# Portions of one lane pair's output between the scores of the next, in a recurrent attention kernel

## The reference

```python
def _attn_ref(r, k, v, w, u):          # B, H, S, D = 2, 8, 768, 48
    state = zeros((B, H, D, D))
    for t in range(S):
        kt, vt, rt, wt = k[:, :, t], v[:, :, t], r[:, :, t], w[:, :, t]
        cur = einsum('bhd,bhe->bhde', u[None] * kt, vt)
        y[:, :, t] = einsum('bhd,bhde->bhe', rt, state + cur)
        state = wt[:, :, :, None] * state + einsum('bhd,bhe->bhde', kt, vt)
    return y
...
x = attn_out.transpose(0, 2, 1, 3).reshape(B, S, H * D)
X = fft(fft(x, axis=1), axis=2);  u = x + real(X)
un = (u - mean(u)) / sqrt(var(u) + 1e-06)
x = u + maximum(un @ w_ch1, 0) @ w_ch2
...                                     # then a gated block with w_in, w_sg, w_out
```

## Time and profile before

| | us |
|---|---|
| median of 3 runs | 447.88 |
| lowest, highest | 446.8, 449.64 |
| the profiled execution | 449.1 |
| its span, first to last instruction | 447.0 |
| TensorE busy in the span | 411.4 (92%) |
| VectorE, ScalarE, GpSimd busy | 257.8, 164.7, 155.2 |

### The profile page before, as it was taken

How to read it: one execution, slowest core, us unless ns; L and a number is a source line. 1 busy time by engine, 2 the same in 40 slices (tenths; PEclk the granted TensorE clock), 3 DMA queues, 4 the chain that set the end, 5 groups by cost and what they waited for, 6 DMA issues and landing times.

```text
span 447.0 us, 10469 instructions
## 1 busy us (share of the span) xinstructions
PE 411.4 (92%) x4352; PEld 390.6 (87%) x4352; DVE 257.8 (58%) x520; ACT 164.7 (37%) x333; POOL 155.2 (35%) x173
## 2 busy tenths in 40 slices
PE   1767977989999999999998999999999999999997
PEld 1756867979998989989988999999899999899997
DVE  4969566788543386352565234211689574598562
ACT  3688245435522566222312112112357121456110
POOL 2989202779900464004202166500007010016000
PEclk9989796989999999999999999999999999999999
DMA  8990018384221300000007755200000002000002
GB/s 261 417 384 10 3 18 326 86 304 111 72 81 59 130 1 4 1 1 1 1 0 244 285 142 145 69 0 1 0 1 0 1 1 77 31 1 0 1 17 89
DMA packets 10702, 37.80 MB, mean 85 GB/s; under 512 B 1440, under 2 KB 3232, under 8 KB 9888
## 3 DMA queue, kind: packets, MB, share of 16 engines
q1 hardware_dynamic: 9648, 24.16, 16.8%
q0 software_dynamic: 1008, 12.99, 7.3%
HBM read 34.78 MB, written 2.36 MB: 83 GB/s over the span
## 4 chain that ended last, share of the span: by engine, by line
PE 66%; issue 15%; POOL 9%; DVE 5%; ACT 3%; DMA 1%; SPq 0%; POOLq 0%; DVEq 0%; ACTq 0%
PE PS L1218 19%; PE PS L1220 18%; PE PS L1219 18%; PE PS L1246 4%; POOL R L489 3%; PE PS L1300 3%; POOL WP L474 2%; DMA R<-r_dram 1%; POOL W1L L505 1%; PE PS L1311 1%; PE PS L1398 1%; DVE KW L877 1%; PE PS L1278 1%; DVE UN L1005 1%; DVE UTL L1010 1%
## 5 line engine op out<-in xcount | busy, mean ns | idle before, releaser
L1047 DVE SCALAR_TENSOR_TENSOR HL<-PS,HH 128x384 fp32r<-128x384 f32 x48 | 26.7, 557 | 94.0 <-ACT HH L745 94.0
L745 ACT ACTIVATE HH<-PS 128x384 fp32r<-128x384 f32 x48 | 23.6, 492 | 101.3 <-PE PS L1220 101.3
L1218 PE MATMUL PS<-UTH,W1H 128*128 128x384 f32 x144 | 50.7, 352 | 2.9 <-DVE UTL L1010 2.9
L1218 PE MATMUL PS<-W2H,HH 128*128 128x384 f32 x144 | 50.3, 349 | 0.0
L1220 PE MATMUL PS<-UTH,W1L 128*128 128x384 f32 x144 | 48.9, 340 | 0.0
L1219 PE MATMUL PS<-UTL,W1H 128*128 128x384 f32 x144 | 48.9, 340 | 0.0
L1220 PE MATMUL PS<-W2H,HL 128*128 128x384 f32 x144 | 48.7, 338 | 0.0
L1219 PE MATMUL PS<-W2L,HH 128*128 128x384 f32 x144 | 48.6, 337 | 0.0
L489 POOL TENSOR_TENSOR R<-R,WP 128x384 f32<-128x384 f32 x40 | 39.4, 987 | 9.5 <-ACT UR L659 4.3
L877 DVE TENSOR_TENSOR KW<-KW,WP 128x384 f32<-128x384 f32 x40 | 32.1, 804 | 12.1 <-PE PS L1246 11.6
L1220 PE MATMUL PS<-SGH,ZL 128*128 128x384 f32 x96 | 32.1, 334 | 0.0
(11 more groups left out here) (143 smaller groups left out, 1023.4 us busy)
## 6 DMA issues: line engine op xcount, KB each, us to landing
KW<-kw_dram SPq DMA_DIRECT2D x6, 768.0 KB, 6.2
RAW<-w_dram SPq DMA_DIRECT2D x12, 384.0 KB, 3.3
R<-r_dram SPq DMA_DIRECT2D x8, 384.0 KB, 5.8
V<-v_dram SPq DMA_DIRECT2D x8, 288.0 KB, 6.9
W1H<-w_dram POOLq DMA_DIRECT2D x1, 2304.0 KB, 9.7
W2H<-w_dram POOLq DMA_DIRECT2D x1, 2304.0 KB, 10.0
SGH<-w_sgt_dram POOLq DMA_DIRECT2D x1, 2304.0 KB, 12.6
RAW<-w_sgt_dram SPq DMA_DIRECT2D x6, 384.0 KB, 3.3
```

Source lines behind the costliest of these rows:

```text
L745: act.activation(HH[:, f % HSLOT, :], hidden_bank(n, f), ACT.Relu).then_inc(s_hh, 1)
L1047: dve.scalar_tensor_tensor(HL[:, f % HSLOT, :], hidden_bank(n, f), 0.0, HH[:, f % HSLOT, :].bitcast(F32), ALU.max, ALU.subtract).then_inc( ...
L1218: pe.matmul(dst, lh, rh, start=start, stop=False)
```

## The change

There are three edits. On TensorE, at levels 3 to 5 of pass two, each half portion of the outputs of pairs 0 and 1 is put behind one lane's score instead of behind both: a phase of `within` at levels 3 and 4, an `across` at level 5. With that `across(0)` moves from level 4 to level 5. The store of pair 3's output moves from VectorE to ScalarE. The `token_pairs` calls for pairs 2 and 3 together become calls for pair 2 and for pair 3, and the counts in `s_tf` that the folds wait for are raised by the two further calls.

```diff
@@ POOL fold
-                pool.wait_ge(s_tf, 8)
+                pool.wait_ge(s_tf, 10)
@@ ACT
             store_y(2)
+            store_y(3)
@@ DVE
-            def store_last_y():
-
-                col = 3 * PW
-                dve.wait_ge(s_y, 4)
...
@@ DVE fold
-                dve.wait_ge(s_tf, 4 if g else 3)
+                dve.wait_ge(s_tf, 6 if g else 5)
@@ DVE
-            store_last_y()
-            token_pairs(2, 4, 0)
+            token_pairs(2, 3, 0)
+            token_pairs(2, 3, 1)
+            token_pairs(3, 4, 0)
             fold(0, 0)
-            token_pairs(2, 4, 1)
+            token_pairs(3, 4, 1)
@@ PE, pass two
             for lev in range(NLEV):
                 for q in range(2, 4):
                     score(q, lev)
+                    if lev in (3, 4):
+                        within(lev - 3, q - 2)
+                    if lev == 5:
+                        across(q - 2)
...
-                if lev == 4:
-                    across(0)
-                if lev in (3, 4):
-                    within(lev - 3, 0)
-                    within(lev - 3, 1)
-
-            across(1)
+
             transpose_k(2)
```

## The result

| | before | changed |
|---|---|---|
| median, 12 runs each | 448.29 us | 449.65 us |
| lowest, highest | 446.43, 449.64 | 448.52, 451.06 |
| ratio to before, 95% interval | | 1.0038 [1.0021, 1.0055] |
| the profiled execution, its span | 449.1, 447.0 | 449.6, 447.5 |

The change makes the kernel slower by 0.38%, 1.7 us with an interval of 0.9 to 2.5. That is inside 1%, and the interval leaves out no change. The forecast was 448.0 us, +0.1 us: the time lies in its range of 446.2 to 450.3, the shift of 1.7 us lies beyond its bounds of 0.0 to +0.95, which the interval just touches.

What follows compares the result with a forecast made beforehand. TensorE's work from 45.3 and the chain to the transform at 69.88 were taken as the bound; +0.53 for the order and -0.43 for the hand-over gave +0.1, 447.88 to 448.0 us, range 446.2 to 450.3.

Steps and rivals of the forecast that it cites:

- What bounds the kernel: From 45.3 to the transform at 69.88, one chain of waiting steps; TensorE itself bounds 45.32 to 55.69, 10.37 us.
- rival (3): First `within` phase: the 0.82 us idle was no wait for a state, so the phase fills it; 446.0 us, chance 0.05.
- its milder form: TensorE ahead of the first `within`: scores pass the waiting phase; 447.2 us, chance 0.02.
- Part one, the order: TensorE, levels 3 to 5: moved score less saved waits, +0.53 us, bounds +0.45 and +1.28.
- the moved score: Pair 3's score of level 3 moves from idle into the stretch TensorE bounds: +0.78 us, upper bound 1.28.
- the waits: Second phases of `within` no longer directly follow the first, for whose end they wait: -0.25 us, bounds 0 and -0.33.
- rival (2): TensorE's score costs its full 1.28 us, no phase gives anything back, the hand-over gains nothing; 449.2 us, chance 0.13.
- the return at 50.4: TensorE's clock goes from half to full at 50.40 in either order, so no added half-clock cost.
- rival (1): TensorE's clock returns one step later, 3.4 us more at half clock, costing 1.7 us; 449.7 us, chance 0.12.
- its own sign: In the changed profile, TensorE's clock would come back to full behind 52.
- Part two, the hand-over: Last `across` to the fold: copy on ScalarE saves 0.12, shorter token sum 0.31; -0.43 us, bounds -0.33 and -0.45.
- The slack of 0.06 us: Pair 2's two token sums on VectorE end at 65.70, just before pair 3's store at 65.76, so they are hidden.

Runs made afterwards that it cites:

- e7: Changed kernel with idle matmuls, results unread: 6 ahead of pair 2's score of level 3, 10 behind it; 447.48 us, ratio 1.0002.
- e8: Kernel before with idle matmuls, results unread: 6 ahead of pair 2's score of level 3, 4 behind pair 3's; 446.62 us, ratio 0.9971.
- e10: Kernel before, unchanged, run once more for a second trace; 448.39 us.
- e6: Changed kernel with the opposite TensorE order: four `within` phases together behind level 3's scores, both `across` behind level 4; 445.83 us, ratio 0.9968.
- e2: Changed kernel with TensorE's old order, so only the new store and token sums remain; 447.44 us, ratio 0.9982.
- e3: Kernel before with the new TensorE order at levels 4 and 5 only, no score blocked; 447.64 us, ratio 1.0006.
- e11: Changed kernel, run once more for a second trace; 450.79 us.
- e12: Kernel before with the new TensorE order at level 3 only, run once more for a trace; 449.02 us.
- e4: Kernel before with the new TensorE order at level 3 only, levels 4 and 5 as before; 449.60 us, ratio 1.0030.

## Why the prediction was right, and where it was not

**What bounds the kernel.** Right. The first phase starts at 45.0 to 45.4 in every trace used here, whatever stands around it, and the whole path behind it moves with it. The reading of the "issue" as a wait for pair 0's last state holds: rival (3), in which the phase would fill the idle, did not happen, nor did its milder form. The score behind the blocked phase stood still until 46.79, although its keys were ready before the 43.23 at which it ran in the earlier trace rows; TensorE did nothing in the 2.51 us between. The rule that was weighed, of the Trainium skill, "TensorE: Matmul & The Clock Gate", section "Step-by-step: what each phase is for", that matmuls stay in program order, is borne out by that 2.51 us.

**Part one, the order.** Here a term was mis-sized. The forecast took +0.78 for the moved score and -0.25 for the waits, and said of five more changes of shape that the trace showed no price, since 48.35 and 50.82 followed without a gap. At equal clock the whole is +1.03 (e7 less e8), against +0.53 forecast. Its parts can be read from e10, e7 and e6. A group followed by one of its own shape takes 0.70 from start to start, one followed by another shape 0.83 to 0.85, one whose successor waits for its end 0.96. The old stretch has five changes of shape and two waits, the new one eleven changes, the last being that to the transposes: 0.70 for the score, six changes at 0.14, two waits less at 0.26, together +1.02. The price was in the earlier trace rows all along: 48 records of score in 1.55 us are 0.70 and 0.85, not two of 0.775. The rows overlap there, and an overlap hides a price as well as a gap would show one. The forecast also counted five further changes, one too few, as rival (2) did.

**The half clock.** The forecast took the return at 50.4 as the same in both orders, and gave rival (1), in which TensorE stays at half clock longer, a chance of 0.12. What the runs showed is neither. The single profiled execution of before had 5.10 us at half clock in the stretch, where four of the six comparable traces had 0.1 or none (e10, e2, e3, e6). The forecast read a matter of the single execution as a property of the kernel, and put a change of the half clock at nothing. With a blocked score it was there in all four unfilled traces, for 1.25 us more on average than without. Rival (1) looked at the right thing, TensorE longer at half clock, but not by its own sign: the clock was back at 50.74, 50.04, 49.06 and 48.79 in the four, never behind 52. Its price of 1.7 us for 3.4 us at half clock is 1.5 by the 0.43 measured here. The half clock of before is also why the two profiled executions lie only 0.57 us apart at the transform: the one of before had its half clock at this place as well.

**Part two, the hand-over.** Right: -0.43 forecast, -0.40 in the idle ahead of the transform, in every trace. The fold started 1.21 us after the last `across` (67.29 less 66.08, where the fourth output released the queue's next load), 1.18 forecast. The slack of 0.06 us did not quite hold: the three token sums ran without a gap from 66.06, so the second of pair 2, and not the store of pair 3 that ended at 66.73, set the start of the third. That cost a few hundredths of a microsecond.

**Sum.** +0.1 forecast, +1.7 measured. The range and the 1% class held because all terms are small against both; that is no merit of the sum. The sum had the order 0.5 us too low and nothing at all for the half clock, and its bounds of 0.0 to +0.95 were missed, as were two signs, the transposes at 56.1 to 56.3 (56.89) and the transform within 0.3 of 69.9 (70.45). The range of the likeliest case, 447.0 to 449.1, did not take in 449.65 either. The forecast's 1% was also not the limit of what can be told: the interval is 0.8 us to each side. Rival (1) came nearest in time with 449.7, by luck in the size. Rival (2), 449.2, was right in part: it held the alternation against the change, but denied the hand-over its gain.

**What stays open.** Between the transposes near 95 us and the next ones near 150, single executions of both orders take more than the 54.2 us of most traces. In e2, e10 and e11 it is 1.5 to 1.6 us more, and each of these has a stretch of 3.4 us at half clock there, from 139.04, 139.60 and 142.20, which by the 0.43 is worth 1.5. In e7 it is 2.7 us more with no half clock behind 99.2, and that is unexplained: single VectorE operations there take 1.5 us that take 0.17 in e8 (the means at 102.25). Whether the change shifts how often either happens was not tried; it may be part of the 1.4 us between e7 and e8. Open too is how the block brings the half clock, as said above.

## What to carry to other kernels

Put a group of matmuls behind a wait only if nothing that is ready stands behind it: a ready score behind a phase that waits costs its own time (0.70 us here), and the longer idle can cost as much again through the clock (1.25 us here, roughly). To price a change of order among small matmuls, take the start-to-start time of one group with each kind of successor (0.70, 0.84, 0.96 here), not the mean over a run of equal groups. And before a term is built on a stretch at half clock in one profile, take a second profile: the same kernel had 5.10 us of it in one execution and none in another.

## What the runs showed of the hardware

- The length of the half-clock stretch depends on the single execution. The same list took 8.21 us in two traces (e2, e10) and 10.37 in a third (before). What TensorE did before it fell differed: in the changed kernel nothing for 1.09 us, in before a score since 43.23 with 0.43 us of idle ahead of it, in e12 a score for 0.23 us with 1.71 us of idle ahead of it. In e7, busy for 4.99 of 5.06 us there, it did not fall.
- Idle matmuls can pay. Ten of them for the kernel before, whose results nobody reads, gave 0.9971 [0.9954, 0.9988].
- Alternating shapes cost about 0.14 us for each change at full clock (0.83 to 0.85 us a group against 0.70). At half clock a score took 1.48 and a phase 1.45 us with another shape behind it.
- One execution of e4 out of 12 took 802 us. In its profile the median 128x384 matmul of the first feed-forward block (`UTH`, L1218) lasts 550 ns, where the profile of before has 338, and a phase and a score near 50 us step by 1.47 and 1.48 us as at half clock, while the record of the granted clock says 1.00 there and between 100 and 700 us. The Trainium skill, "TensorE: Matmul & The Clock Gate", section "Seeing it yourself", warns that on this chip the clock's records have been unreliable; this trace agrees.
